# A second layer-1 square per chunk as a fast three-part product, and the work around it moved between ScalarE and GpSimd

## What is computed

```python
def _moe_ref(x, w_in, w_out):          # layer 1
    h = x @ w_in
    r = np.maximum(h, 0.0)
    g = r * r
    return g @ w_out

def _moe2_ref(x, w_in, w_out, a, b):   # layer 2
    h = x @ w_in
    h2 = h * h
    h3 = h2 * h
    P = a[0] + a[1] * h + a[2] * h2 + a[3] * h3
    Q = 1.0 + np.abs(b[0]) * np.abs(h) + np.abs(b[1]) * h2
    g = P / (Q + 1e-06)
    return g @ w_out
```

## Time and profile before

| | |
|---|---|
| median of three runs | 1517.66 us |
| the profiled execution | 1517.89 us, its span 1515.9 us |
| TensorE (PE) busy | 1483.7 us, 98% |
| VectorE (DVE) busy | 1445.2 us, 95% |
| ScalarE (ACT) busy | 1378.8 us, 91% |
| GpSimd (POOL) busy | 1248.3 us, 82% |
| chain that ended last | PE 88%, DVE 5%, ACT 2%, POOL 2% |
| granted TensorE clock | 1.0 |

### The profile page before, as it was taken

How to read it: one execution, slowest core, us unless ns; L and a number is a source line. 1 busy time by engine, 2 the same in 40 slices (tenths; PEclk the granted TensorE clock), 3 DMA queues, 4 the chain that set the end, 5 groups by cost and what they waited for, 6 DMA issues and landing times.

```text
span 1515.9 us, 20584 instructions
## 1 busy us (share of the span) xinstructions
PE 1483.7 (98%) x5576; PEld 991.1 (65%) x5576; DVE 1445.2 (95%) x2549; ACT 1378.8 (91%) x2672; POOL 1248.3 (82%) x1225
## 2 busy tenths in 40 slices
PE   5999999999999999999999999999999999999988
PEld 4999999765666666666666666666666666666655
DVE  7888888889999999999999999999999999999998
ACT  3777777689999999999999999999999999999997
POOL 4544445359999999999999999999999999999897
PEclk9999999999999999999999999999999999999999
DMA  6200001000000000000000000000000000000000
GB/s 224 84 21 28 21 27 43 1 1 1 8 8 8 1 8 8 8 8 1 7 8 8 0 8 8 8 1 8 7 8 1 8 8 8 8 1 8 8 8 7
DMA packets 11518, 24.21 MB, mean 16 GB/s; under 512 B 1440, under 2 KB 2336, under 8 KB 11168
## 3 DMA queue, kind: packets, MB, share of 16 engines
q1 hardware_dynamic: 11424, 23.14, 4.5%
HBM read 16.85 MB, written 6.29 MB: 15 GB/s over the span
## 4 chain that ended last, share of the span: by engine, by line
PE 88%; DVE 5%; ACT 2%; POOL 2%; issue 1%; DMA 1%; SPq 0%; POOLq 0%; ACTq 0%; DVEq 0%
PE psum L937 19%; PE psum L974 18%; PE psum L801 11%; PE psum L800 11%; PE psum L802 11%; PE psum L889 6%; PE psum L852 6%; PE psum L874 4%; DVE tb L727 1%; DVE tb L736 1%; DVE tb L753 1%; DVE g1h L713 1%; DVE psum L741 1%; POOL tb L410 1%; DMA X<-kvT 1%
## 5 line engine op out<-in xcount | busy, mean ns | idle before, releaser
L412 POOL TENSOR_TENSOR wb<-wb,ub 128x512 f32<-128x512 f32 x384 | 496.4, 1293 | 29.4
L937 PE MATMUL psum<-tb,wout 128*128 128x512 f32 x736 | 375.8, 592 | 2.5 <-DVE tb L785 2.3
L974 PE MATMUL psum<-g,wout 128*128 128x512 f32 x690 | 352.4, 592 | 0.2 <-ACT x2f L528 0.2
L404 POOL TENSOR_SCALAR wb<-ub,babs 128x512 f32<-128x512 f32 x384 | 296.0, 771 | 35.5 <-ACT ub L550 30.3
L800 PE MATMUL psum<-x2h,win2h 128*128 128x512 f32 x384 | 283.3, 738 | 2.6 <-POOL x2l L397 2.5
L727 DVE SCALAR_TENSOR_TENSOR tb<-tb,ca,psum 128x512 f32<-128x512 f32 x364 | 267.8, 736 | 4.6 <-ACT psum L584 4.5
L736 DVE SCALAR_TENSOR_TENSOR tb<-tb,ca,psum 128x512 f32<-128x512 f32 x365 | 269.6, 739 | 0.0
L551 ACT ACTIVATE tb<-psum,ca 128x512 f32<-128x512 f32 x384 | 267.1, 696 | 0.0
L550 ACT ACTIVATE ub<-psum 128x512 f32<-128x512 f32 x384 | 233.0, 607 | 23.5 <-PE psum L802 23.5
L568 ACT ACTIVATE lnb<-wb 128x512 f32<-128x512 f32 x384 | 248.3, 647 | 5.2 <-POOL wb L412 4.8
L753 DVE SCALAR_TENSOR_TENSOR tb<-psum,tb 128x512 f32<-128x512 f32 x364 | 248.1, 682 | 2.6
(11 more groups left out here) (109 smaller groups left out, 2506.6 us busy)
## 6 DMA issues: line engine op xcount, KB each, us to landing
qraw<-qT SPq DMA_DIRECT2D x23, 256.0 KB, 2.6
outT<-osb SPq DMA_DIRECT2D x23, 256.0 KB, 2.0
X<-kvT SPq DMA_DIRECT2D x15, 384.0 KB, 7.7
wraw<-w_in SPq DMA_DIRECT2D x2, 1024.0 KB, 8.3
X<-kvT SPq DMA_DIRECT2D x2, 192.0 KB, 10.5
outT<-osb SPq DMA_DIRECT2D x2, 128.0 KB, 1.8
qraw<-qT SPq DMA_DIRECT2D x1, 192.0 KB, 10.2
wsr<-w_sr SPq DMA_DIRECT2D x1, 64.0 KB, 1.8
```

The source lines that it names most:

```text
L404: nc.gpsimd.tensor_scalar(w, u, babs[:, 1:2], babs[:, 0:1], ALU.mult, ALU.add).then_inc(v_rdy, 1)
L412: nc.gpsimd.tensor_tensor(w, w, u, ALU.mult).then_inc(w_rdy, 1)
L937: mm(ACC2, wout2[:, f, :], tb[:, t % T_RING, :], start=(f == 0), stop=(f == NF - 1))\
L974: mm(ACC1, wout1[:, f, :], g1[:, t % G_RING, :], start=(f == 0), stop=(f == NF - 1))\
```

## The change

Four things, all in the feed-forward part:

1. `SPLIT_COLS` becomes (5, 13): column 5 is halved too, in chunks 1 to 23. ScalarE computes its g1h (in step 6), GpSimd its g1l, and TensorE's `out1` of it goes through `three`.
2. The full square of column 13 goes from GpSimd to ScalarE, right behind g1h of the same tile in step 14.
3. GpSimd's g1l of column 13 comes a step later, in step 14, behind that step's L404 and L412 (L405 and L413 in the changed file); g1l of column 5 stands in step 5, behind the square.
4. x1's two parts, both at the head of step 5 before, stand at the head of step 6 (x1h) and of step 8 (x1l).

```diff
         def on_act(t):
-            return t < NF or t % 2 == 0
-        SPLIT_COLS = (13,)
+            return t < NF or t % 2 == 0 or t % NF in (13,)
+        SPLIT_COLS = (5, 13)
...
         def squares_act(t):
-            return t + 1 if t < NF else NF + (t - NF) // 2 + 1
+            return sum(on_act(x) for x in range(t + 1))
         def squares_pool(t):
-            return max(0, (t - NF + 1) // 2)
+            return sum(not on_act(x) for x in range(t + 1))
...
             for s in range(STEPS):
-                if s % NF == 5 and 1 <= s // NF < NCH - 1:
+                if s % NF == 6 and 1 <= s // NF < NCH - 1:
                     x1_high(s // NF + 1)
+                if s % NF == 8 and 1 <= s // NF < NCH - 1:
                     x1_low(s // NF + 1)
...
                     nc.gpsimd.tensor_tensor(g1[:, t % G_RING, :], r, r, ALU.mult).then_inc(sqp_rdy, 1)
-                    if halved(t):
-                        n = halves(t)
-                        pool.wait_ge(sqh_rdy, n + 1)
-                        pool.wait_ge(sqp_rdy, squares_pool(t))
-                        nc.gpsimd.tensor_tensor(g1l[:, n % 2, :], g1[:, t % G_RING, :], g1h[:, n % 2, :].bitcast(F32),
-                                                ALU.subtract).then_inc(sql_rdy, 1)
+                t = s - 1
+                if halved(t) and on_act(t):
+                    n = halves(t)
+                    pool.wait_ge(sqh_rdy, n + 1)
+                    pool.wait_ge(sqa_rdy, squares_act(t))
+                    nc.gpsimd.tensor_tensor(g1l[:, n % 2, :], g1[:, t % G_RING, :], g1h[:, n % 2, :].bitcast(F32),
+                                            ALU.subtract).then_inc(sql_rdy, 1)
+                t = s
+                if halved(t) and not on_act(t):
...
+                    pool.wait_ge(sqp_rdy, squares_pool(t))
+                    nc.gpsimd.tensor_tensor(g1l[:, n % 2, :], g1[:, t % G_RING, :], g1h[:, n % 2, :].bitcast(F32),
+                                            ALU.subtract).then_inc(sql_rdy, 1)
...
                     nc.scalar.activation(g1h[:, n % 2, :], r1[:, t % R_RING, :], ACT.Square).then_inc(sqh_rdy, 1)
+                    if on_act(t):
+                        nc.scalar.activation(g1[:, t % G_RING, :], r1[:, t % R_RING, :],
+                                             ACT.Square).then_inc(sqa_rdy, 1)
                 t = s - 1
-                if in_b(t) and on_act(t) and s != LAG:
+                if in_b(t) and on_act(t) and not halved(t) and s != LAG:
```

## The result

The changed kernel takes 1541.17 us (median of five runs, 1539.52 to 1541.98) against 1517.74 us for the kernel before beside it (1517.64 to 1518.15). The ratio is 1.015, with a 95% interval of 1.0137 to 1.0164. It was forecast at 1544.1 us, between 1532 and 1552. Its profiled execution took 1541.98 us with a span of 1540.2 us, 24.1 us more than before's 1517.89.

A forecast was written before the change was run, and what follows sets the result against it. PE was taken to set the pace at 49.66 us a chunk, three engines close behind. 22 chunks at 1.35 - 0.16 = 1.19 give 26.2 us, with chunk 23 26.4: 1544.1 us median, range 1532 to 1552.

The forecast's parts named there:

- PE gains 0.16 us by halving a column: Column 5's step on PE takes 2.95 us instead of 3.11, in 23 chunks: 3.7 us if nothing waits.
- POOL falls behind from step 5 to 10, ACT's L568 waits in steps 7, 9 and 11: POOL's work there is about 2 us too long; L568 waits 0.3, 0.8 and 0.3 us.
- ub of step 14 comes late behind two squares, g1l(13) behind that, and PE stands: ub at 751.92, g1l ending at 756.01; PE's column 13 `out1` in step 15 waits, in chunks 1 to 22.
- The size of the pause: PE stands 1.35 us in each of chunks 1 to 22, net 1.19 after the 0.16 gained: 26.2 us.
- The price of the late release: In step 15, PE's first matmul ends 0.56 us after g1l ends; with nothing there, 12.3 us less, 1532.
- Chunk 1 like the others: Chunks 1 to 22 were each given the full net cost of 1.19 us.
- the pauses lower the clock: Rival: after each pause PE runs a step at the lower clock, 68 us more, about 1612; chance 0.01.
- Chunk 23: No x1 there, so POOL catches up: a pause of 0.33 us, net 0.17.
- Hidden altogether: Rival: PE keeps its pace at 49.50 a chunk and gains 3.7 us, 1514.0; chance 0.07.
- The two squares alone: Rival: POOL's backlog does not matter, every chunk is like the last, 3.9 us more, 1521.6; chance 0.07.
- ScalarE as the bound by its sum: Beside the two-squares rival: ACT's 48.67 + 1.07 = 49.74 us a chunk, 1519.5; within that rival's chance of 0.07.
- More than one pause: Rival: x2l in step 2 or VectorE late for `out2` adds 0.3 us a chunk or more, beyond 1552; chance 0.04.

The follow-up runs named there:

- Number 7: Kernel before with column 5 halved too and only x1l moved, to the head of step 9: 1517.7 us, ratio 0.9999.
- Numbers 3: Kernel before with only x1's parts moved, from step 5 to steps 6 and 8: 1518.08 us, ratio 1.0.
- 4: Changed kernel with both of x1's parts at the head of step 13 in place of steps 6 and 8: 1522.59 us, ratio 1.0031.
- Number 2: Kernel before with only column 13's full square moved to ScalarE and its g1l to step 14: 1525.73 us, ratio 1.0052.
- number 8: Changed kernel with x1's parts at the head of step 13 in chunk 1 only: 1538.93 us.
- 9: Second trace of the kernel before with column 5 halved too and only x1l moved, to step 9: 1515.66 us, one execution.
- number 6: Changed kernel with x1's parts at the head of step 13 and g1l of column 13 at the head of step 14: 1517.07 us, ratio 0.9996.
- number 5: Changed kernel with g1l of column 13 ahead of L405 and L413 in step 14, x1 left in place: 1534.06 us, ratio 1.0108.

## Why the prediction was right, step by step

**PE gains 0.16 us by halving a column: right.** Number 7 shows it where nothing waits, 49.49 against 49.65.

**POOL falls behind from step 5 to 10, ACT's L568 waits in steps 7, 9 and 11: right, place by place.** In the trace after POOL's L405 of step 5 waits for ub, and the next wait is behind step 11. ACT waits 0.68 us by the row of step 9, and about 0.2 in steps 7 and 11 (L580 stands at 741.62 and 754.50, each 1.28 behind its ub, where its own spacing is 1.06). The forecast had 0.8, 0.3 and 0.3. Numbers 3 and 4 show what it takes: x1's place costs nothing by itself, and 18.6 us with the rest of the change.

**ub of step 14 comes late behind two squares, g1l(13) behind that, and PE stands: right.** Number 2 shows its own share, 0.36 us a chunk, without any backlog.

**The size of the pause: 1.35 us forecast, 1.12 measured.** Net 1.19 against 0.945 a chunk. This is the mis-sized term, and it is in the spacings on POOL that I carried over. In the earlier trace rows x1h to x1l is 0.69 and L404 to L412 0.86, because the second reads what the first has just written. Where the next instruction is another one, it follows sooner: x1h to L405 0.60 (738.86 to 739.46), and L405 to L411 0.74 (751.19 to 751.93), since L411 does not read L405's result. With 0.03 less behind g1l and 0.02 less behind the square ahead of x1l, that is 0.09 + 0.12 + 0.03 + 0.02 = 0.26 us a chunk, and 1.19 less 0.26 is 0.93. The pair in which both times a square is followed by the same kind of instruction says the same: 1.18 to g1l, which reads it, and 1.00 to x1l, which doesn't (743.67 to 744.67). The price of the late release held: g1l ended at 766.86, the matmul at 767.48, 0.62 against 0.56. The rest cancels: from L580 of step 11 to ub of step 14 it is 0.08 less than forecast, from there to the end of the matmul 0.10 more.

Two readings in the prediction are off, and its walk uses neither. g1l of column 13 was there 1.92 us early, not over two (703.01 to 704.93). And POOL's net growth is 0.24, not 0.40, since the square that left took 1.18 ahead of its g1l and not 1.02.

**Chunk 1 like the others: wrong.** It costs 3.8 us, not 1.19. It starts without `out2` in its first steps, ScalarE has no spare time in it (number 8), and PE is idle for 1.94 us ahead of g1h's product, where the same row of a later chunk has 0.87. Behind that pause the clock fell. PE and the windows of the kernel after:

```profile
355.00:358.00 3.00, 3.00 (x11) 1.71 (x10) 3.00 (x6) 3.00 (x7) 1.44 (x3) 1.00 0.00 0
358.00:360.50 2.50, 0.61 (x2) 0.00 (x0) 2.50 (x5) 2.50 (x7) 2.50 (x3) 1.00 0.00 0
...
362.00:364.00 2.00, 2.00 (x6) 1.56 (x5) 2.00 (x4) 1.55 (x4) 2.00 (x3) 0.50 0.00 0
```

```profile
360.55 0.47 PE L812 MATMUL psum<-g1h,wo1h 128*128 128x512 f32 x1 [1.94 <-POOL g1l L425]
...
361.90 0.63 PE L814 MATMUL psum<-x2h,win2l 128*128 128x512 f32 x1
362.33 0.63 PE L812 MATMUL psum<-x1h,win1h 128*128 128x512 f32 x1
...
363.61 1.74 PE L949 MATMUL psum<-tb,wout 128*128 128x512 f32 x2
365.18 1.02 PE L986 MATMUL psum<-g,wout 128*128 128x512 f32 x2
```

The granted clock is 0.50, the 1.2 GHz level, from about 361.7 to 365. Matmuls that follow each other every 0.23 us do so every 0.43 (361.90 to 362.33), and L949 takes 1.57 to its successor in place of 0.86. Four of the one and one of the other make 0.8 + 0.7 = 1.5 us. Counted to the end of the product, as the 1.12 of the later chunks, the pause is 2.19 us (357.59 to 361.02 is 3.43, less 1.24). Together with the 1.5, and less the 0.16 gained, that is 3.5 of the 3.8. This is the rival "the pauses lower the clock", in one chunk of 22. It did not hold for the others: behind a pause of 1.12 us the clock is 1.00. The Trainium skill (TensorE: Matmul & The Clock Gate, "What's actually happening") says that the clock is set by how busy PE was just before; the two cases agree with it, and number 8, with 1.54 us of idle time in chunk 1 and the clock up, does too. But the length of the pause alone does not decide it. The same trace has a second low stretch, from 1484.6 to 1488.0, behind 1.89 us of idle time, which costs nothing (57.70 us from the last x2l to the end, and 57.69 in number 8 without it); the kernel before has 2.20 us of idle time at that place and stays at 1.00, and numbers 7 and 9, one kernel, differ there. So 1.5 of the 24.1 us are of a kind that one execution has and another may not.

**Chunk 23: right within 0.3 us.** +0.17 was forecast, and the last x2l shows 24.22 us against 24.33 one chunk earlier. The pause is there, 0.38 us (L949 at 1473.44, the product's end at 1475.06) for 0.33 forecast. That the chunk is 0.11 shorter even so is not explained.

**The rivals.** Hidden altogether: refuted (49.50 a chunk needed). The two squares alone: numbers 2 and 4 show them as a third of it. ScalarE as the bound by its sum: its busy 49.63 of 50.59 and number 6, which has all of ScalarE's new work at 49.57 a chunk, refute it. More than one pause: refuted for the later chunks, where PE's wait for g1l is the only one of PE in the list; chunk 1 has a small second one, 0.31 us for VectorE's L765 at 340.10.

The prediction's total of 26.4 us is 2.3 above the profiled execution's 24.1: 21 chunks at 0.945 in place of 1.19 are 5.1 less, chunk 23 is 0.3 less, and chunk 1 and the start are 3.3 more; 0.2 are left over. That the total came nearer than its parts is luck: the mis-sized pause and the missed cost of chunk 1 go opposite ways.

## What to carry to other kernels

Where several engines are each above 93% busy in the part that repeats, a sum over the whole does not tell enough: lay the new lists on the old clock and walk from the step in which everyone last waited for the leader to the next one. Ask of each added instruction what stands right behind it on its engine, and of each moved one whether it leaves a place with spare time; here two instructions of 1.9 us that stand behind a wait made four fifths of the loss together with the new g1l, and nothing by themselves (numbers 3 and 4). And a delay that is taken off one place goes on to the next (number 5), so look for the second place before taking off the first.

## What was not expected of the hardware

Of two GpSimd instructions in a row, the second starts 0.60 us after the first's start where it is independent, and 0.69 where it reads the first's result (x1h, 0.61 us long); for L405 of 0.78 us it is 0.74 against 0.86, and for a square of 1.05 us 1.00 against 1.18. On TensorE, 1.94 us of idle time in chunk 1 were followed by a low clock that cost 1.5 us more, while the pauses of the 21 later chunks, 0.87 us in the same reading, cost nothing more than themselves. And two executions of one kernel differ in whether the clock falls at one and the same place: 0.50 and 1.00 behind 2.39 and 2.36 us of idle time.
